# Top-k mask of attention: scores folded into halves, mask added on GpSimd before the exponential, ELU in one VectorE operation

## The reference

```python
# q, k, v: (4, 8, 576, 64)
scores = (1 / sqrt(64)) * q @ k^T                   # 4 x 8 x 576 x 576
kth    = the 32nd largest score of each row
scores = where(scores >= kth, scores, -1e9)
attn   = exp(scores - rowmax); attn /= attn.sum(-1) + 1e-9
x      = (attn @ v) as 2304 x 512
# dense network: w_in 512 x 2048, w_out 2048 x 512
h = x @ w_in
g = where(h > 0, h, exp(min(h, 0)) - 1)             # ELU
x = g @ w_out
# mixture: 8 experts, w1 512 x 1024, w2 1024 x 512, each token goes to one expert
logits = cosine(x, expert_emb) / tau; expert = argmax; gate = softmax weight
out = gate * (relu(x @ w1[expert]) @ w2[expert])
```

## Time and profile before

| | |
|---|---|
| median of 3 runs | 1390.48 us |
| profiled execution, time / span | 1388.3 / 1386.6 us |
| TensorE (PE) busy, share of span | 1213.3 us, 88% |
| VectorE (DVE) busy | 932.9 us, 67% |
| ScalarE (ACT) busy | 543.0 us, 39% |
| GpSimd (POOL) busy | 247.0 us, 18% |
| mean granted TensorE clock | 0.931 |

### The profile page before, as it was taken

One profiled execution on the slowest core, in us unless ns is written; L12 is line 12 of the kernel. 1 busy time (PEld: TensorE's weight loads), 2 busy tenths in 40 slices (PEclk: granted clock), 3 DMA queues, 4 the chain that ended last, 5 costly groups with the idle time before them and its releaser, 6 DMA issues.

```text
span 1386.6 us, 21604 instructions
## 1 busy us (share of the span) xinstructions
PE 1213.3 (88%) x7809; PEld 937.1 (68%) x7810; DVE 932.9 (67%) x2320; ACT 543.0 (39%) x1243; POOL 247.0 (18%) x391
## 2 busy tenths in 40 slices
PE   3656666799999999999999999999984999999996
PEld 2444444586787786687777677797864777677773
DVE  4999999999999999999999999610226110011100
ACT  3433443574474565465466456251620000000000
POOL 0212111140151042033023024000000111111111
PEclk9866666799999999999999999999996999999998
DMA  3141100100100100001011000000160354415100
GB/s 112 37 142 48 26 17 10 27 10 18 32 21 18 44 10 18 23 22 27 9 36 26 10 13 7 1 18 0 48 230 16 119 188 157 150 64 214 69 32 21
DMA packets 80121, 72.48 MB, mean 52 GB/s; under 512 B 60310, under 2 KB 60310, under 8 KB 79520
## 3 DMA queue, kind: packets, MB, share of 16 engines
q1 hardware_dynamic: 73584, 56.13, 12.9%
q0 software_dynamic: 3760, 10.49, 2.3%
q10 hardware_dynamic: 2688, 4.72, 1.2%
HBM read 61.88 MB, written 11.27 MB: 53 GB/s over the span
## 4 chain that ended last, share of the span: by engine, by line
PE 52%; DVE 36%; issue 5%; ACT 3%; POOL 2%; DMA 0%; SPq 0%; DVEq 0%; ACTq 0%; POOLq 0%
DVE work L848 15%; DVE top L844 14%; PE mlp L543 12%; PE sc L643 11%; PE pv_ps L653 10%; PE mlp L534 8%; DVE probs L859 5%; PE pv_ps L515 3%; PE sc L486 3%; PE tp L494 1%; POOL g L398 1%; PE mlp L552 1%; PE tp L623 1%; PE prep_ps L559 1%; POOL elu_e L396 1%
## 5 line engine op out<-in xcount | busy, mean ns | idle before, releaser
L844 DVE MAX8 top<-work 128x8 f32<-128x576 f32 x432 | 310.1, 744 | 0.1
L543 PE MATMUL mlp<-g,wout 128*128 128x288 f32 x1024 | 270.0, 411 | 0.0
L543 PEld LDWEIGHTS mlp<-g,wout 128*128 128x128 f32 x1024 | 187.7, 190 | 61.9 <-issue 17.4
L848 DVE MATCH_REPLACE8 work<-top,work 128x576 f32<-128x576 f32 x288 | 213.0, 740 | 0.0
L698 ACT COPY probs_t<-tp 128x640 f32<-128x640 f32 (+1 forms) x144 | 108.3, 752 | 191.2 <-PE tp L498 151.7
L494 PE MATMUL tp<-ident,probs 128*128 128x128 f32 x720 | 117.5, 300 | 59.0 <-DVE probs L859 59.0
L534 PE MATMUL mlp<-x_h,win_h 128*128 128x288 f32 x512 | 162.5, 317 | 0.1
L643 PEld LDWEIGHTS sc<-xg_t,w_exp 128*128 128x128 f32 x1344 | 154.6, 193 | 11.3 <-issue 11.3
L643 PE MATMUL sc<-xg_t,w_exp 128*128 x1344 | 154.9, 276 | 1.3 <-ACT act_tick L807 1.3
L534 PE MATMUL mlp<-x_h,win_l 128*128 128x288 f32 x512 | 151.5, 296 | 0.0
L534 PE MATMUL mlp<-x_l,win_h 128*128 128x288 f32 x512 | 151.5, 296 | 0.0
(11 more groups left out here) (159 smaller groups left out, 1400.5 us busy)
## 6 DMA issues: line engine op xcount, KB each, us to landing
w_exp<-in_moe_w SPq DMA_DIRECT2D x16, 2048.0 KB, 13.7
x_rows<-g ACTq DMA_DIRECT2D x24, 192.0 KB, 2.1
raw_qk<-in_q SPq DMA_DIRECT2D x32, 128.0 KB, 2.4
raw_qk<-in_k SPq DMA_DIRECT2D x32, 128.0 KB, 2.4
vals<-in_v SPq DMA_DIRECT2D x32, 128.0 KB, 2.3
g<-in_moe_w_in SPq DMA_DIRECT2D x4, 1024.0 KB, 5.3
wout<-in_moe_w_out SPq DMA_DIRECT2D x1, 4096.0 KB, 15.9
raw_qk<-in_q SPq DMA_DIRECT2D x32, 16.0 KB, 2.2
```

Source lines behind the costliest of these rows:

```text
L543: mm = pe.matmul(mlp_ps[bank_][:, 0:HS], wout[:, c, i * P:(i + 1) * P], g[:, c * HS:(c + 1) * HS], start=(c == 0), stop=(c == FC - 1))
L844: chain.mark(dve.max(top[:, T % 2, 8 * r:8 * r + 8], src))
L848: chain.mark(dve.match_replace(out=w_, in_to_replace=top[:, T % 2, 8 * r:8 * r + 8], in_values=scores[:, T % NSC, :] if r == 0 else w_, im ...
```

## The change

- **Top-k.** For each tile the row's two halves of 288 columns are folded: `larger` (VectorE) writes the elementwise maximum, `both_halves` (GpSimd) the integer sum of the bit patterns, and `smaller` (GpSimd) subtracts the maximum's bits from the sum, which leaves the smaller of each pair. The 32 largest of the first list (four `eight`, three `without`) and the 16 largest of the second (two `eight`, one `without`) are found over 288 columns each. `meet` and `threshold` combine the sorted lists to the 32nd largest: the largest of min(first[15+i], second[15-i]) and first[31].
- **Mask.** On GpSimd, ahead of the exponential: `probs` = (scores < threshold) * -1e30, then `probs` += scores. The exponential then reads `probs` in place and sums the row on ScalarE.
- **ELU.** relu(-h) and exp go to `g` in place; VectorE writes max(g - 1, h), reading h from PSUM, in the loop and after it. The bank is free only after that.
- **Order.** `LAG` 7 and `XT` 4 for 6 and 3; `turn` and its copy are three slots behind, `expo` two; scores are made two slots ahead; the preparation of the next pair moves from positions 3 to 5 to positions 5, 6 and the end of 6; `q_t` has one buffer.

```diff
-    LAG = 6
+    LAG = 7
-        XT = 3
+        XT = 4
 # gpsimd
+            def both_halves(T):
+                wait(pool, sc_evac, scores_of(T))
+                wait(pool, thr_done, T - 2)
+                s_ = scores[:, T % NSC, :].bitcast(I32)
+                pool.tensor_tensor(work[:, T % 3, 1, :].bitcast(I32), s_[:, 0:HS], s_[:, HS:S], ALU.add).then_inc(summed_up, 1)
+            def smaller(T):
+                wait(pool, summed_up, T + 1)
+                wait(pool, larger_done, T + 1)
+                m_ = work[:, T % 3, :, :].bitcast(I32)
+                pool.tensor_tensor(m_[:, 1, :], m_[:, 1, :], m_[:, 0, :], ALU.subtract).then_inc(folded, 1)
-            def elu(mb, m, pos):
...
+            def mask(T):
+                pr = probs[:, T % 2, 0:S]
+                wait(pool, thr_done, T + 1)
+                wait(pool, tr_done, T - 1)
+                pool.tensor_scalar(pr, scores[:, T % NSC, :], thr[:, T % 2:T % 2 + 1], -BIG, ALU.is_lt,
+                                   ALU.mult).then_inc(dropped, 1)
+                wait(pool, dropped, T + 1)
+                pool.tensor_tensor(pr, scores[:, T % NSC, :], pr, ALU.add).then_inc(mask_done, 1)
             for s in range(END):
-                if 0 <= s - 2 < NT and ends_group(s - 2):
-                    widen(group_of(s - 2))
+                if 0 <= s - 2 < NT:
+                    mask(s - 2)
+                if s + 1 < NT:
+                    both_halves(s + 1)
+                if 0 <= s - 3 < NT and ends_group(s - 3):
+                    widen(group_of(s - 3))
+                if s + 1 < NT:
+                    smaller(s + 1)
 # tensor
             def turn(T):
-                wait(pe, mask_done, T + 1)
+                wait(pe, exp_done, T + 1)
             def mlp(mb, m, pos):
...
-                        wait(pe, mlp_free[bank_], BANK_USES[bank_] * mb + n)
+                        wait(pe, mlp_free[bank_], ACT_USES[bank_] * mb + by_act)
+                        wait(pe, g_done, FC * 2 * mb + chunk if chunk else 0)
 # scalar
             def expo(T):
+                wait(act, mask_done, T + 1)
+                act.activation(probs[:, T % 2, 0:S], probs[:, T % 2, 0:S], ACT.Exp, bias=..., scale=SCALE,
+                               accum_out=rowsum[:, G % 2, head_of(T):head_of(T) + 1]).then_inc(exp_done, 1)
             def mlp(mb, m, pos):
+                        act.activation(at, mlp_ps[bank_][:, 0:HS], ACT.Relu, scale=-1.0).then_inc(elu_neg, 1)
-                        act.activation(g[:, i * HS:(i + 1) * HS], mlp_ps[bank_][:, 0:HS],
-                                       ACT.Relu).then_inc(mlp_free[bank_], 1)
+                        act.activation(at, at, ACT.Exp, scale=-1.0).then_inc(elu_exp, 1)
 # vector
+            def larger(T):
+                wait(dve, sc_evac, scores_of(T))
+                dve.tensor_tensor(work[:, T % 3, 0, :], scores[:, T % NSC, 0:HS], scores[:, T % NSC, HS:S],
+                                  ALU.max).then_inc(larger_done, 1)
+            def meet(T):
+                chain.mark(dve.tensor_tensor(lists[:, MEET], lists[:, TOP_K // 2 - 1:TOP_K - 1],
+                                             lists[:, 2 * TOP_K - 1:3 * TOP_K // 2 - 1:-1], ALU.min), ("meet", T))
+            def threshold(T):
+                dve.tensor_reduce(thr[:, T % 2:T % 2 + 1], top[:, T % 2, TOP_K - 1:3 * TOP_K // 2],
+                                  AX_X, ALU.max).then_inc(thr_done, 1)
-            def mask(T):
...
             def slot(s):          # new order; until() waits for the named instruction
+                eight(new, 0, 0); total(summed); without(old, 0, 1)
+                larger(s + 1); reciprocal(summed); eight(old, 0, 2)
+                wait(dve, folded, new + 1); without(new, 0, 0); without(old, 0, 2)
+                mlp(step of s - 1, second position)
+                eight(new, 1, 0); eight(old, 0, 3); eight(new, 0, 1); meet(old); bias(old)
+                without(new, 1, 0); threshold(old); normalise(weighed); eight(new, 1, 1)
+                mlp(step of s, first position)
             def mlp(mb, m, pos):
+                        dve.scalar_tensor_tensor(out=at, in0=at, scalar=-1.0, in1=mlp_ps[i % 2][:, 0:HS],
+                                                 op0=ALU.add, op1=ALU.max).then_inc(g_done, 1)
```

More of the change, by code:

```diff
@@ L567, in _ @@
             for c in range(KD):
[L568 removed]
+                last = pe.transpose(mlp_ps[0][:, c * E:(c + 1) * E], work[0:E, 0, :, :].rearrange("p a n -> p (a n)")[:, c * P:(c + 1) * P], ident[0:E, 0:E])
             last.then_inc(emb_tr, 1)
@@ L578, in _ @@
                 p, t = divmod(s, PT_)
-                if 3 <= t < 6 and p + 1 < NP:
-                    prep(p + 1, t - 3)
-                G = group_of(s) + 1 if s < NT else NP * GP
-                if starts_group(s) and G < NP * GP:
+                if t in (5, 6) and p + 1 < NP:
+                    prep(p + 1, t - 5)
+                G = scored_in(s)
+                if G is not None:
                     score(G, 0)
@@ L585, in _ @@
                     mlp(*step, 0)
-                back = s - 2
+                if G is not None:
+                    score(G, 1)
+                back = s - 3
                 if 0 <= back < NT:
                     turn(back)
-                if ends_group(s) and G < NP * GP:
-                    score(G, 1)
                 if step:
@@ L664, in prep @@
                 if r == 0:
-                    act.copy(q_t[:, p % 2, :], prep_ps[:, 0:FULL * P]).then_inc(prep_evac, 1)
+                    wait(act, sc_half, SP_ * (p - 1) + 4 * FULL if p else 0)
+                    act.copy(q_t[:, :], prep_ps[:, 0:FULL * P]).then_inc(prep_evac, 1)
                 elif r == 1:
@@ L712, in row, with mlp @@
                 return g[0:R, FC * HS - (RB - i) * DM:FC * HS - (RB - 1 - i) * DM]
-            def mlp(mb, m, pos, last):
-                for kind, blk, i, part, parts, n in mlp_at(m, pos):
+            def mlp(mb, m, pos):
+                for kind, blk, i, part, parts, n, _ in mlp_at(m, pos):
                     bank_ = 0 if kind == "rows" else i % 2
@@ L838, in _ @@
             chain = Chain()
-            def eight(T, r):
-                src = scores[:, T % NSC, :] if r == 0 else work[:, T % 2, :]
-                chain.mark(dve.max(top[:, T % 2, 8 * r:8 * r + 8], src))
-            def without(T, r):
-                w_ = work[:, T % 2, :]
-                chain.mark(dve.match_replace(out=w_, in_to_replace=top[:, T % 2, 8 * r:8 * r + 8],
-                                             in_values=scores[:, T % NSC, :] if r == 0 else w_, imm_value=NEG))
-            def bias(T):
-                dve.tensor_scalar(negmax[:, T % 2:T % 2 + 1], top[:, T % 2, 0:1], -SCALE, None,
-                                  ALU.mult).then_inc(rowmax, 1)
@@ new lines, in _, with ranked, eight @@
+            MEET = slice(TOP_K, 3 * TOP_K // 2)
+            def ranked(T, half, r):
+                lo = RANKS[half].start + 8 * r
+                return top[:, T % 2, lo:lo + 8]
+            def larger(T):
+                wait(dve, sc_evac, scores_of(T))
+                dve.tensor_tensor(work[:, T % 3, 0, :], scores[:, T % NSC, 0:HS], scores[:, T % NSC, HS:S],
+                                  ALU.max).then_inc(larger_done, 1)
+            def eight(T, half, r):
+                chain.mark(dve.max(ranked(T, half, r), work[:, T % 3, half, :]), ("eight", T, half, r))
@@ new lines, in without @@
+            def without(T, half, r):
+                w_ = work[:, T % 3, half, :]
+                chain.until(("eight", T, half, r))
+                chain.mark(dve.match_replace(out=w_, in_to_replace=ranked(T, half, r), in_values=w_, imm_value=NEG),
+                           ("without", T, half, r))
+            def bias(T):
+                chain.until(("eight", T, 0, 0))
+                wait(dve, exp_done, T - 1)
+                chain.mark(dve.tensor_scalar(negmax[:, T % 2:T % 2 + 1], top[:, T % 2, 0:1], -SCALE, None, ALU.mult),
+                           ("bias", T))
@@ L892, in slot @@
                 old = s - 1 if 0 <= s - 1 < NT else None
-                summed = group_of(s - 2) if 0 <= s - 2 < NT and ends_group(s - 2) else None
-                weighed = group_of(s - 3) if 0 <= s - 3 < NT and ends_group(s - 3) else None
+                summed = group_of(s - 3) if 0 <= s - 3 < NT and ends_group(s - 3) else None
+                weighed = group_of(s - 4) if 0 <= s - 4 < NT and ends_group(s - 4) else None
                 if new is not None:
-                    wait(dve, sc_evac, scores_of(new))
-                    eight(new, 0)
+                    wait(dve, larger_done, new + 1)
+                    eight(new, 0, 0)
                 if summed is not None:
```

189 lines of the change are left out of this document (102 added, 87 removed).

## The result

The changed kernel takes 1476.8 us (median of four runs, 1474.81 to 1479.1) where the kernel before takes 1390.33: a ratio of 1.0622, 95% interval 1.0604 to 1.0641. The prediction said 1403 with a range up to 1460, so its sign was right and its size was 74 us short: it forecast 12.5 us of loss, and the measured loss is seven times that. The profiled execution has a span of 1473.1 us.

A forecast was written before the change was run, and what follows sets the result against it. VectorE set the slot before; afterwards a ring through VectorE and GpSimd was to bind. First stage -4.5 us, second +11.4, after the loop +5.6: +12.5 on the profiled 1388.3, 1403 us against the runs' median, range 1335 to 1460.

The forecast's parts named there:

- VectorE's own work: VectorE's instructions on 288 columns: 0.37 us a MAX8, 0.43 a load with replace; 4.72 us a slot, 5.46 in hidden slots.
- The integer operations at 0.80, the add at 1.41: GpSimd's two integer operations over 288 columns take 0.80 us each, the mask's add over 576 columns 1.41 us.
- The comparison at 0.67: GpSimd's compare-and-multiply for the mask over 576 columns takes 0.67 us, bounds 0.67 to 1.41.
- Rival 3: GpSimd's compare is slow, anywhere up to 1.41 us: up to 107 us more in all, halfway 1456 us; chance 12%.
- the ring: Turn through both engines: threshold, GpSimd's compare and add, `larger` waiting for the add, next threshold; 5.56 us, 5.93 with hidden chunk.
- not the trouble: GpSimd's throughput: its work of 4.2 us a slot fits, if barely, into VectorE's 4.72.
- about 1470: Time if GpSimd's compare were an estimated 0.5 us longer, from the skill's 2.03 cycles an element against 1.03.
- rival 1: `larger` gets through the port at once: first-stage slots some 4.9 us, second stage at TensorE's 5.68, 1324 us; chance 25%.
- Rival 2: GpSimd's queued integer add takes the port before waiting `larger`: 0.75 us more in some 65% of slots, 1473 us; chance 13%.
- have a slot to themselves: Exponential behind the mask and the transpose each get a whole slot, one slot of lag more each, so they are hidden.
- The weight splits at 0: Eight weight splits ahead of GpSimd's mask: up to 2 us each later, `larger` saves up to 0.8; taken as 0.
- The sign: Whole kernel: slower 55%, faster 38%, the same 7%; 0.9% slower forecast.

## Why the prediction was wrong

- **VectorE's own work**: right. MAX8, replace and `larger` have the forecast durations.
- **The integer operations at 0.80, the add at 1.41**: right (0.797 and 1.413).
- **The comparison at 0.67**: the step that failed. It takes 2.21 us, outside the bounds of 0.67 to 1.41. The row it went by, a compare-and-fill of 0.28 over 128 columns, is another instruction, and the upper bound came from adds; neither holds for a comparison with a scalar. Rival 3 named the mechanism, but with too small a size and the wrong price: the length isn't added to the ring, it dissolves the ring and makes GpSimd's queue (2.21 + 1.41 + 0.80 + 0.80 and waits, 5.7 us where 4.2 was counted) the bound ahead of the network. The prediction had called GpSimd's throughput "not the trouble". By the last matmul the length costs 34.4 us, or 28.2 when the preparation is early. The estimate that the prediction worked out from the Trainium skill, "GPSIMD Engine Reference", section "Performance pitfalls for Q7 kernels", was 0.5 us more for a comparison; the runs show 1.5. Its time of about 1470 came close by luck: the price per slot was three times too small, and it was added to a ring that isn't there.
- **The ring through the port**: right where the comparison is short, in the turns without a split or a change of pair (5.6, 6.0, 6.8). In the changed kernel it doesn't exist. The signs that the prediction gave led astray: `larger` at 0.45 was to mean rival 1 and a faster kernel; it came together with a slower one. The sign of rival 3, a compare of over 1 us, pointed right.
- **Rival 2**: refuted, 1.01 us for the integer sum that had to wait.
- **The exponential and the transpose "have a slot to themselves"**: wrong where the network runs and one pair follows another. The comparison waits 92 us for the transposes of the tile two before it. The moved preparation was named among the edits and given no price; it costs 25 to 29 us in the changed kernel, 13 to 19 with the comparison short.
- **The weight splits at 0**: not borne out. Its bounds were -6 and +16 us. With the fold they cost 12 us in a kernel near this one. Within the changed kernel itself no run took them away; there they are 27.9 us (8 x 3.49) of the 254.2 for which GpSimd is busy in the 284.8 us up to the network's first matmul.
- **The sign** came out as forecast, but mostly through terms that the sum didn't have: 12.5 of the 84.9 us by which the last matmul is late were in it.

The sum, by the last matmul: 12.5 forecast, 34.4 for the comparison, 19.3 for the preparation (with the comparison short), and 18.7 that no run gives to one cause: 84.9. In the other order it is 25.5 for the preparation and 28.2 for the comparison. Of the 18.7 some 17 lie ahead of the network, where slots took 6.14 us with both taken away and 5.73 was forecast (42 x 0.41). There stand the splits, and `total`, which waits over 0.5 us for the port in 15 of its 22 uses there, where half was counted. What each of them is worth stays open.

## What to carry to other kernels

Price an operation on GpSimd by a row of the same operation, not of the same shape; where there is none, a row of another instruction gives no upper bound. When work is folded to make one engine's slot shorter, count how many two-input operations then meet on VectorE and GpSimd and in which order they are released: kernels with the same fold ran from 6.2% slower to 1.5% faster here, by what triggered the sum, who had the mask and the ELU, when the next pair was prepared and how long the split's pieces were. In a queue that is nearly full, look for the rare long pieces: here eight splits of 3.5 us. And price each moved step at the place where its users change over, not in the average slot.

## What the runs showed of the hardware

- GpSimd, 128 x 576 in float32 with a scalar operand: comparison with multiply 2.21 us, subtract with minimum 2.24, add with multiply 0.75, multiply with add in place 0.67. VectorE makes the comparison in 0.50.
- The 2.21 us comparison holds VectorE's two-input operation back for about its first 0.7 us, a two-input add for its whole 1.41.
- `larger`, waiting on VectorE for GpSimd's add to end, goes ahead of the integer sum that GpSimd starts next (1.01 us for 0.79).
- VectorE's operation over 16 columns waits as long as one over 288: 2.35 us for 0.15. An operation with one input and two columns waits too (`total`, up to 2.01 us).
- TensorE's granted clock fell to 0.50 for 17.1 us at each of two changes of pair of the changed kernel (533.2 and 765.3 us), after TensorE had been busy 93% of the 14.7 us in front of the first; with the pair prepared earlier it stayed at 1.00 at both places.
